# Two PSUM banks of a unit in one VectorE instruction, in a kernel of chunked gated attention and two MLPs

## The chip, the cores and the metric

One core of one Trainium2 chip runs the whole program. The metric is device time in microseconds. Times come from several executions of each kernel; one further execution is profiled.

## The reference

```python
for t in range(S):                       # 768 steps, batch 4, 8 heads, head size 40
    m_new = max(f_gate + m, i_gate)
    f_stab, i_stab = exp(f_gate + m - m_new), exp(i_gate - m_new)
    C = f_stab * C + i_stab * outer(v, k)
    n = f_stab * n + i_stab * k
    denom = max(abs(n . q), 1.0)
    y[t] = sigmoid(o_gate) * (C @ q) / denom
x = y as (3072 tokens, 320)
h = x @ w_in;   x = max(0.01 * h, h) @ w_out        # 320 -> 2048 -> 320
h = x @ w_in2;  out = (h * cos(h)) @ w_out2         # the same sizes
```

All data is float32 in DRAM. The MLP products are made from a rounded high part and a remainder, three matmuls for each product of two.

## The kernel before, in words

The recurrence is cut into **units**: one batch and one chunk of 128 tokens, 24 units in all, each with two sub-chunks of 64. The MLPs go over eight **blocks** of 384 tokens, three units each. The MLPs' hidden layer is 16 tiles wide, and a tile of one block is a **slot** of the program: in it TensorE (PE) makes eight matmuls of 384 columns for the hidden tile (`first_product`, L698) and nine matmuls of 320 columns for the output sums of an earlier tile (`second_product`, L711 to L713). The order of all work is written out by hand. While the first MLP works on block n, the slots also carry the attention work of the three units of block n + 1, at places fixed by the tables `FIRST_SLOTS` and `UNIT_SLOTS` (`SCORES`, `PROBS`, `STATE`, `OUTPUTS`, `READ`, `TURN`, ...). The first three units run before the first slot. In the second MLP no attention work is left.

A unit uses two PSUM banks, one for each half of its heads. After the first three units (which use `s0` and `s1`, then `h0` and `h1`, then `acc0` and `acc1`) these are always `s0` and `s1`. Its path is this:

- PE makes the scores into columns 0 to 255 of both banks (L617).
- VectorE (DVE) multiplies them with the decays `D` (`probs`, L1159; for the first three units `first_probs`, L1168), one instruction for each bank, 128 x 256 each.
- PE makes the unit's own part of the state (`unit_state`, L637). It waits for `P_done` of this unit's probabilities and for `x1_done` of the unit before.
- DVE adds the state up (`state`, L1254 and L1246). GpSimd (POOL) masks it (`own_state`, L1462).
- PE makes the outputs and the sums for the normaliser (`unit_within` L667, `unit_carried` L652).
- DVE makes the normaliser `max(|n.q|, 1)` and its reciprocal (`normaliser`, L1190, L1194, L1197): `max(-x, 1)` and then `max(x, .)`, each in one instruction for each bank, 128 x 4 each, then one reciprocal over all eight heads. `nrm_done` releases POOL, which multiplies the gate with it (`gated`, L1470).
- DVE multiplies outputs and gate (`outputs`, L1227 and L1228 for the last 64 columns, L1231 for all of them, one instruction for each bank, 128 x 160 each). Unit 2 alone has its outputs normalised in PSUM first (`normalised`, L1204).
- PE transposes the result (`unit_transpose`, L674). ACT rounds it (L871) and DVE takes the remainder (`x_lo`, L1264, L1265).

POOL runs in its own written order. For each unit: `gated` of the unit before (L1470), `decay_logs` (L1432), `mask` (L1437), `keys` (L1449), `carried` (L1443), then `own_state` (L1462). So whatever releases L1470 sets the start of the four instructions behind it.

In every slot of the first MLP, DVE also takes the maximum of the leaky ReLU (L1288) and the remainder of the hidden tile (`g_rest`, L1273), which reads two tensors of SBUF. The order on DVE in a slot is: normaliser, probabilities, state, L1288, L1273, outputs, `x_lo`, sigmoid reciprocals (L1150), remainder of a turned block.

During the first block the weights of the first MLP are also loaded and split into high and low parts. ACT rounds (`copy`, L871), DVE or POOL subtracts (DVE L1364; POOL L1526, L1557), and the loads wait for the buffers that these free.

Of the kernel before, what the change touches and what calls it, by code (L numbers as in the profile page):

```python
# [20 lines left out]
F32 = mybir.dt.float32  # L21
F32R = mybir.dt.float32r
ALU = mybir.AluOpType
ACT = mybir.ActivationFunctionType

P = 128
BATCH, HEADS, SEQ, HD = 4, 8, 768, 40
CHUNK = 128
# [4 lines left out]
TILES = BLOCK // P  # L33
DM, FF = HEADS * HD, 2048
# [3 lines left out]
SIDE = HEADS // 2  # L38
PACK, GROUPS = 2, 4
VD = HD + 1  # L40
# [5 lines left out]
BUFS = 3  # L46
# [37 lines left out]
def build(nc, qk, q3, kvo, ig, fg, w1i, w1o, w2i, w2o, out, g_dram, e_dram, x2_dram):  # L84
    ctx = ExitStack()
    with ctx:
        def sb(name, shape, dt=F32):
            return ctx.enter_context(nc.sbuf_tensor(name, shape, dt))

        def bank(name):  # L90
            return ctx.enter_context(nc.psum_tensor(name, [P, 512], F32))

        def sem(name):
            return ctx.enter_context(nc.semaphore(name))
# [18 lines left out]
        D = sb("D", [P, BUFS, SIDE, CHUNK])  # L113
# [34 lines left out]
        m_s = [g_f[0:GH, 0, :], g_f[0:GH, 1, :]]  # L148
        G_s = [t_f[0:GH, 0, :], t_f[0:GH, 1, :]]

        acc = [bank(f"acc{t}") for t in range(TILES)]
        h_bank = [bank("h0"), bank("h1")]
        s_bank = [bank("s0"), bank("s1")]
        x_bank = bank("x")
        ring_bank = h_bank + s_bank

        gates_in = sem("gates_in")
# [423 lines left out]
        def first(b, c):  # L581
            return isinstance(b, int) and b == 0 and c < TILES

        def unit_banks(b, c):
            return (s_bank, h_bank, acc[0:2])[c] if first(b, c) else s_bank

        def scale_bank(c):
            return (h_bank[0], acc[0], x_bank)[c]
# [503 lines left out]
        def _(dve):  # L1092
# [59 lines left out]
            def probs(b, c):  # L1152

                dve.wait_ge(O_done, unit(b, c))
                dve.wait_ge(S_done, unit(b, c) + 1)
                dve.wait_ge(D_done, late(b, c))
                for e in range(2):
                    d = D[:, c % BUFS, 2 * e:2 * e + 2, :]
                    last = tt(d, unit_banks(b, c)[e][:, 0:2 * CHUNK].rearrange("p (h t) -> p h t", h=2), d, ALU.mult)  # L1159
                last.then_inc(P_done, 1)  # L1160

            def first_probs(c):

                dve.wait_ge(S_done, c + 1)
                dve.wait_ge(dx_done, c + 1)
                for e in range(2):
                    d = D[:, c, 2 * e:2 * e + 2, :]
                    last = tt(d, unit_banks(0, c)[e][:, 0:2 * CHUNK].rearrange("p (h t) -> p h t", h=2), d, ALU.mult)  # L1168
                last.then_inc(ph_done, 1)

            def first_keys():

# [4 lines left out]
                   kn_s[:, 0, :, :].rearrange("p (u h) d -> p u h d", u=SUBS), weights.to_broadcast([P, SUBS, SIDE, HD]),  # L1177
                   ALU.mult).then_inc(kw0_done, 1)

            def output_heads(b, c, e):  # L1180
                return unit_banks(b, c)[e][:, OUT:OUT + SIDE * VD].rearrange("p (h d) -> p h d", h=SIDE)

            def normaliser(b, c):

                n, p = unit(b, c), c % 2
                dve.wait_ge(O_done, n + 1)
                sums = [output_heads(b, c, e)[:, :, HD] for e in range(2)]
                parts = [nrm[:, p, SIDE * e:SIDE * (e + 1)] for e in range(2)]
                for o, x in zip(sums, parts):
                    last = ts(x, o, -1.0, 1.0, ALU.mult, ALU.max)  # L1190
                last.then_inc(nrm_step, 1)
                dve.wait_ge(nrm_step, n * 2 + 1)
                for o, x in zip(sums, parts):
                    last = tt(x, o, x, ALU.max)  # L1194
                last.then_inc(nrm_step, 1)
                dve.wait_ge(nrm_step, n * 2 + 2)
                nc.vector.reciprocal(nrm[:, p, :], nrm[:, p, :]).then_inc(nrm_done, 1)  # L1197

            def normalised(b, c):

                dve.wait_ge(nrm_done, unit(b, c) + 1)
                for e in range(2):
                    o, x = output_heads(b, c, e)[:, :, 0:HD], nrm[:, c % 2, SIDE * e:SIDE * (e + 1)]
                    last = tt(o, o, x.unsqueeze(2).to_broadcast([P, SIDE, HD]), ALU.mult)  # L1204
                last.then_inc(normed_done, 1)

            def by_gate(b, c):

# [2 lines left out]
            def outputs(b, c):  # L1211

                p = c % 2
                if by_gate(b, c):
                    dve.wait_ge(gated_done, unit(b, c) + first(b, c))
                else:
                    dve.wait_ge(normed_done, 1)
                    dve.wait_ge(sig_done, 2 * unit(b, c) + 2)
                gate = o_s[:, c % BUFS, :].rearrange("p (h d) -> p h d", h=HEADS)
                if first(b, c):  # L1220
                    if c == 2:
                        dve.wait_ge(T_done, 1)
                else:
                    h, d = divmod(2 * P, HD)
                    n = HD - d
                    o = output_heads(b, c, 1)
                    tt(x1[:, p, DM:DM + n], o[:, h - SIDE, d:HD], gate[:, h, d:HD], ALU.mult)  # L1227
                    tt(x1[:, p, DM + n:DM + REM], o[:, h + 1 - SIDE, 0:HD], gate[:, h + 1, :], ALU.mult)  # L1228
                for e in range(2):
                    heads = slice(SIDE * e, SIDE * (e + 1))  # L1230
                    last = tt(x1[:, p, 0:DM].rearrange("p (h d) -> p h d", h=HEADS)[:, heads, :],  # L1231
                              output_heads(b, c, e)[:, :, 0:HD], gate[:, heads, :], ALU.mult)
                last.then_inc(x1_done, 1)

            def state(b, c):

# [430 lines left out]
```

## Time and profile before

| | us |
|---|---|
| median of 3 runs | 818.16 |
| lowest, highest run | 818.14, 820.23 |
| profiled execution | 818.53 |
| its span, first to last instruction | 816.8 |
| PE busy | 805.9 (99%) |
| DVE busy | 631.1 (77%) |
| ACT busy | 466.6 (57%) |
| POOL busy | 347.2 (43%) |

The granted TensorE clock is 1.00 over the whole span, which is the upper one of its two levels. PE has 6953 matmuls, DVE 1371 instructions. Busy time is a share of the span and says nothing yet of who waits for whom; for that the waits and the timeline are read.

### The profile page before, as it was taken

The page shows a single profiled execution, that of the slowest core. Times are in us where ns is not written, and L with a number is a line of the kernel's source. Part 1 is how long each engine was busy: PE and PEld are TensorE (multiplying, and loading weights), DVE is VectorE, ACT ScalarE, POOL GpSimd, SP SyncE. Part 2 cuts the span into 40 slices and gives each one's busy share as a digit, 9 for nine tenths or more (in the row PEclk, how much of TensorE's full clock was granted, in tenths as well). Part 3 has the DMA queues.
Part 4 walks back from the last instruction along what each step waited for, and adds up shares of the span by engine and source line. Part 5 has one row for each costly group of instructions (what it writes and reads, how often), then busy time and mean ns, then how long its engine had stood idle before and what let it go on. Part 6 is the DMA issues. An engine that isn't in the chain of part 4 may idle for free.

```text
span 816.8 us, 18114 instructions
## 1 busy us (share of the span) xinstructions
PE 805.9 (99%) x6953; PEld 782.8 (96%) x6953; DVE 631.1 (77%) x1371; ACT 466.6 (57%) x1037; POOL 347.2 (43%) x350
## 2 busy tenths in 40 slices
PE   8999999999999999999999999999999999999998
PEld 6888999999999999999999999999999999999998
DVE  8889777776777777777644688888888888888896
ACT  5554433443434334434356777777777777777776
POOL 5877553333343534433126543343434343433332
PEclk9999999999999999999999999999999999999999
DMA  9776243323223333240034401210010202020000
GB/s 288 220 201 195 91 123 105 129 80 129 81 93 131 122 104 128 81 144 31 2 116 127 164 2 49 73 50 25 9 65 1 74 1 73 1 73 1 2 24 25
DMA packets 36952, 70.10 MB, mean 86 GB/s; under 512 B 3524, under 2 KB 24068, under 8 KB 36868
## 3 DMA queue, kind: packets, MB, share of 16 engines
q1 hardware_dynamic: 36820, 68.91, 25.9%
q8 instruction: 55, 0.90, 0.5%
q14 instruction: 29, 0.24, 0.1%
q10 hardware_dynamic: 48, 0.05, 0.0%
HBM read 56.95 MB, written 11.99 MB: 84 GB/s over the span
## 4 chain that ended last, share of the span: by engine, by line
PE 88%; DVE 5%; POOL 2%; ACT 1%; issue 1%; DMA 1%; SPq 0%; DVEq 0%; POOLq 0%; ACTq 0%
PE h L698 32%; PE acc L711 13%; PE acc L713 13%; PE acc L712 12%; PE s L698 10%; PE x L674 2%; PE s L637 2%; PE s L652 2%; DVE r_f L1300 2%; PE s L617 2%; PE s L667 1%; DVE r_f L1298 1%; DMA raw_in<-w1i 1%; DVE g_f L1308 0%; POOL w_in L1526 0%
## 5 line engine op out<-in xcount | busy, mean ns | idle before, releaser
L698 PE MATMUL h<-xT,w_in 128*128 128x384 f32 x1536 | 305.9, 341 | 1.4 <-DVE w_in L1364 0.9
L698 PEld LDWEIGHTS h<-xT,w_in 128*128 128x128 f32 x1536 | 266.3, 188 | 5.5 <-DVE w_in L1364 1.1
L871 ACT ACTIVATE t_f<-h 128x384 f32<-128x384 f32 x192 | 94.1, 490 | 280.7 <-PE h L698 280.6
L711 PE MATMUL acc<-w_out,g_hi 128*128 128x320 f32 x756 | 237.1, 314 | 0.7 <-POOL g_lo L1600 0.3
L713 PE MATMUL acc<-w_out,g_lo 128*128 128x320 f32 x756 | 233.6, 309 | 0.0
L712 PE MATMUL acc<-w_out,g_hi 128*128 128x320 f32 x756 | 232.3, 307 | 0.0
L1600 POOL TENSOR_TENSOR g_lo<-g_f,g_hi 128x384 fp32r<-128x384 f32 x123 | 125.9, 1024 | 204.0 <-ACT g_hi L871 204.0
L1288 DVE TENSOR_TENSOR g_f<-h,t_f 128x384 f32<-128x384 f32 x128 | 71.2, 556 | 107.9 <-ACT t_f L871 107.4
L711 PEld LDWEIGHTS acc<-w_out,g_hi 128*128 128x128 f32 x756 | 142.0, 188 | 2.0 <-issue 1.1
L712 PEld LDWEIGHTS acc<-w_out,g_hi 128*128 128x128 f32 x756 | 142.1, 188 | 0.0
L713 PEld LDWEIGHTS acc<-w_out,g_lo 128*128 128x128 f32 x756 | 141.8, 188 | 0.0
L871 ACT ACTIVATE g_hi<-g_f 128x384 fp32r<-128x384 f32 (+1 forms) x254 | 131.0, 516 | 5.1 <-DVE g_f L1308 4.5
L1300 DVE SCALAR_TENSOR_TENSOR r_f<-t_f,r_f 128x384 f32<-128x384 f32 x127 | 117.7, 927 | 4.4
L698 PE MATMUL s<-xT,w_in 128*128 128x384 f32 x512 | 100.8, 338 | 0.0
L1273 DVE TENSOR_TENSOR g_lo<-g_f,g_hi 128x384 fp32r<-128x384 f32 x128 | 90.9, 710 | 0.0
L698 PEld LDWEIGHTS s<-xT,w_in 128*128 128x128 f32 x512 | 89.7, 188 | 0.0
L1010 ACT ACTIVATE r_f<-r_f,half_pi 128x384 f32<-128x384 f32 x127 | 78.5, 618 | 4.1
L1470 POOL TENSOR_TENSOR kvo_s<-kvo_s,nrm 128x320 f32<-128x320 f32 x23 | 16.6, 723 | 147.9 <-DVE nrm L1197 147.9
L1296 DVE TENSOR_SCALAR t_f<-t_f 128x384 f32<-128x384 f32 x127 | 46.6, 367 | 42.3 <-ACT t_f L871 42.2
L1462 POOL TENSOR_TENSOR Cm<-C,own 80x328 f32<-80x328 f32 x44 | 42.9, 979 | 56.1 <-DVE C L1254 45.2
L1008 ACT ACTIVATE r_f<-r_f 128x384 f32<-128x384 f32 x127 | 65.6, 516 | 0.0
L1150 DVE RECIPROCAL kvo_s<-kvo_s 128x160 f32<-128x160 f32 x48 | 54.9, 1144 | 0.0
(160 smaller groups left out, 834.3 us busy)
## 6 DMA issues: line engine op xcount, KB each, us to landing
qk_s<-qk SPq DMA_DIRECT2D x24, 512.0 KB, 4.7
kvo_s<-kvo SPq DMA_DIRECT2D x24, 484.0 KB, 4.9
x_dram<-stage SPq DMA_DIRECT2D x8, 960.0 KB, 4.2
xT<-x_dram SPq DMA_DIRECT2D x8, 960.0 KB, 4.8
D<-g_dram SPq DMA_DIRECT2D x42, 128.0 KB
qe<-q SPq DMA_DIRECT2D x24, 160.0 KB, 3.2
out<-x SPq DMA_DIRECT2D x24, 160.0 KB, 1.8
eG_b<-e_dram SPq DMA_DIRECT2D x42, 80.0 KB
```

The costliest lines, as they stand in the source:

```text
L698: last = nc.tensor.matmul(bank[:, 0:BLOCK], w(a), x[:, k, :], start=(n == 0), stop=(n == 7))
L711: nc.tensor.matmul(acc[t][:, 0:DM], hi[:, r], w_out[:, 0, j, :], start=(j == 0), stop=False)
L712: nc.tensor.matmul(acc[t][:, 0:DM], hi[:, r], w_out[:, 1, j, :], start=False, stop=False)
L713: nc.tensor.matmul(acc[t][:, 0:DM], lo[:, r], w_out[:, 0, j, :], start=False, stop=(j == FT - 1)).then_inc(out_done, 1)
L871: copy = lambda o, i, **k: nc.scalar.activation(o, i, ACT.Copy, **k)
L1008: nc.scalar.activation(r, r, ACT.Abs).then_inc(fold_done, 1)
L1010: nc.scalar.activation(r, r, ACT.Sin, bias=half_pi[:, 0:1], scale=-1.0).then_inc(sin_done, 1)
L1150: nc.vector.reciprocal(o, o).then_inc(sig_done, 1)
L1273: tt(lo_of(row.tile(i)), g_of(row.tile(i)), hi_of(row.tile(i)).bitcast(F32), ALU.subtract).then_inc(lo_done, 1)
L1288: tt(g_of(row.tile(i)), h_bank[i % 2][:, 0:BLOCK], t_f[:, i % 2, :], ALU.max).then_inc(max_done, 1)
L1300: nc.vector.scalar_tensor_tensor(r, k, -TWO_PI_LO, r, ALU.mult, ALU.add).then_inc(red_done, 1)
L1600: nc.gpsimd.tensor_tensor(lo_of(n), g_of(n), hi_of(n).bitcast(F32), ALU.subtract).then_inc(lo_done, 1)
```

## The change

The PSUM banks of `acc`, `h`, `s` and `x` are declared as tensors of several banks. The old names become views of them, so that PE and ACT address what they addressed before. In `probs`, `first_probs`, `normaliser`, `normalised` and `outputs` the loop over the two banks becomes one instruction whose access pattern has a bank dimension. Waits and increments of semaphores stay the same, and the order of what is left stays the same on every engine.

```diff
-        def bank(name):
-            return ctx.enter_context(nc.psum_tensor(name, [P, 512], F32))
+        def banks(name, n):
+            return ctx.enter_context(nc.psum_tensor(name, [P, n, 512], F32))
...
-        acc = [bank(f"acc{t}") for t in range(TILES)]
-        h_bank = [bank("h0"), bank("h1")]
-        s_bank = [bank("s0"), bank("s1")]
-        x_bank = bank("x")
+        acc_banks, h_banks, s_banks, x_banks = banks("acc", TILES), banks("h", 2), banks("s", 2), banks("x", 1)
+        acc = [acc_banks[:, t, :] for t in range(TILES)]
+        h_bank = [h_banks[:, k, :] for k in range(2)]
+        s_bank = [s_banks[:, k, :] for k in range(2)]
+        x_bank = x_banks[:, 0, :]
...
+        def unit_pair(b, c):
+            return (s_banks, h_banks, acc_banks[:, 0:2, :])[c] if first(b, c) else s_banks
...
-                for e in range(2):
-                    d = D[:, c % BUFS, 2 * e:2 * e + 2, :]
-                    last = tt(d, unit_banks(b, c)[e][:, 0:2 * CHUNK].rearrange("p (h t) -> p h t", h=2), d, ALU.mult)
-                last.then_inc(P_done, 1)
+                d = D[:, c % BUFS, :, :].rearrange("p (e h) t -> p e (h t)", e=2)
+                tt(d, unit_pair(b, c)[:, :, 0:2 * CHUNK], d, ALU.mult).then_inc(P_done, 1)
...
-            def output_heads(b, c, e):
-                return unit_banks(b, c)[e][:, OUT:OUT + SIDE * VD].rearrange("p (h d) -> p h d", h=SIDE)
+            def output_heads(b, c):
+                return unit_pair(b, c)[:, :, OUT:OUT + SIDE * VD].rearrange("p e (h d) -> p e h d", h=SIDE)
...
-                sums = [output_heads(b, c, e)[:, :, HD] for e in range(2)]
-                parts = [nrm[:, p, SIDE * e:SIDE * (e + 1)] for e in range(2)]
-                for o, x in zip(sums, parts):
-                    last = ts(x, o, -1.0, 1.0, ALU.mult, ALU.max)
-                last.then_inc(nrm_step, 1)
+                sums, parts = output_heads(b, c)[:, :, :, HD], nrm[:, p, :].rearrange("p (e h) -> p e h", e=2)
+                ts(parts, sums, -1.0, 1.0, ALU.mult, ALU.max).then_inc(nrm_step, 1)
                 dve.wait_ge(nrm_step, n * 2 + 1)
-                for o, x in zip(sums, parts):
-                    last = tt(x, o, x, ALU.max)
-                last.then_inc(nrm_step, 1)
+                tt(parts, sums, parts, ALU.max).then_inc(nrm_step, 1)
...
-                for e in range(2):
-                    o, x = output_heads(b, c, e)[:, :, 0:HD], nrm[:, c % 2, SIDE * e:SIDE * (e + 1)]
-                    last = tt(o, o, x.unsqueeze(2).to_broadcast([P, SIDE, HD]), ALU.mult)
-                last.then_inc(normed_done, 1)
+                o, x = output_heads(b, c)[:, :, :, 0:HD], nrm[:, c % 2, :].rearrange("p (e h) -> p e h", e=2)
+                tt(o, o, x.unsqueeze(3).to_broadcast([P, 2, SIDE, HD]), ALU.mult).then_inc(normed_done, 1)
...
-                for e in range(2):
-                    heads = slice(SIDE * e, SIDE * (e + 1))
-                    last = tt(x1[:, p, 0:DM].rearrange("p (h d) -> p h d", h=HEADS)[:, heads, :],
-                              output_heads(b, c, e)[:, :, 0:HD], gate[:, heads, :], ALU.mult)
-                last.then_inc(x1_done, 1)
+                tt(x1[:, p, 0:DM].rearrange("p (e h d) -> p e h d", e=2, h=SIDE), output_heads(b, c)[:, :, :, 0:HD],
+                   gate.rearrange("p (e h) d -> p e h d", e=2), ALU.mult).then_inc(x1_done, 1)
```

## Rows read from the trace of the kernel before

**Rows 1.** Waits of PE: waited for, us in total, times, longest us
```profile
PE s L637 <- DVE D L1159: 1.5, 1, 1.5
...
PE h L698 <- DVE w_in L1364: 0.9, 1, 0.9
PE s L637 <- issue: 0.7, 1, 0.7
```

**Rows 2.** Busy time by stretch: length, PE, PEld, DVE, ACT, POOL, PEclk, DMA, GB/s
```profile
100.00:150.00 50.00, 49.98 (x484) 47.97 (x483) 37.16 (x99) 19.88 (x45) 21.92 (x21) 1.00 0.35 118
```

**Rows 3.** DVE's groups by form: out, in, count, busy us, mean ns of one
```profile
L1288 DVE TENSOR_TENSOR g_f<-h,t_f 128x384 f32<-128x384 f32 x128 | 71.2, 556 | 107.9 <-ACT t_f L871 107.4
...
L1159 DVE TENSOR_TENSOR D<-s,D 128x256 f32<-128x256 f32 x42 | 15.7, 415 | 0.2
L1231 DVE TENSOR_TENSOR x<-s,kvo_s 128x160 f32<-128x160 f32 x44 | 11.9, 313 | 0.0
...
L1349 DVE TENSOR_TENSOR g_lo<-g_f,g_hi 128x128 fp32r<-128x128 f32 x3 | 0.9, 289 | 1.0 <-ACT g_hi L871 1.0
```

**Rows 4.** Timeline of two units: start us, us, engine, line, idle before
```profile
118.84 0.55 DVE L1273 TENSOR_TENSOR g_lo<-g_f,g_hi 128x384 fp32r<-128x384 f32 x1
...
118.97 1.57 POOL L1437 TENSOR_TENSOR D<-D,hide 128x512 f32<-128x512 f32 x1
...
207.87 0.23 DVE L1190 TENSOR_SCALAR nrm<-s 128x4 f32<-128x4 f32 x2 [0.49 <-PE s L652]
...
208.69 0.72 POOL L1470 TENSOR_TENSOR kvo_s<-kvo_s,nrm 128x320 f32<-128x320 f32 x1 [8.48 <-DVE nrm L1197]
...
210.48 0.55 DVE L1273 TENSOR_TENSOR g_lo<-g_f,g_hi 128x384 fp32r<-128x384 f32 x1
...
210.57 1.61 POOL L1437 TENSOR_TENSOR D<-D,hide 128x512 f32<-128x512 f32 x1
...
211.15 0.55 DVE L1231 TENSOR_TENSOR x<-s,kvo_s 128x160 f32<-128x160 f32 x2
...
211.84 0.43 PEld L674 LDWEIGHTS x<-ident,x 128*128 128x128 f32 x3
```

**Rows 5.** Timeline of the first block where PE waits for L1159
```profile
26.42 0.56 DVE L1231 TENSOR_TENSOR x<-h,kvo_s 128x160 f32<-128x160 f32 x2
...
27.91 3.58 POOL L1526 TENSOR_TENSOR w_in<-raw_in,w_in 128x768 fp32r<-128x768 f32 x2 [1.52 <-DVE t_f L1128]
...
47.93 0.74 DVE L1159 TENSOR_TENSOR D<-s,D 128x256 f32<-128x256 f32 x2
...
48.73 0.81 PE L637 MATMUL s<-kvo_s,kw 64*80 64x82 f32 x16 [1.47 <-DVE D L1159]
```

**Rows 6.** Timeline of the first block, the two units before PE's wait at 72.9
```profile
58.71 0.20 DVE L1197 RECIPROCAL nrm<-nrm 128x8 f32<-128x8 f32 x1
...
71.29 0.72 POOL L1470 TENSOR_TENSOR kvo_s<-kvo_s,nrm 128x320 f32<-128x320 f32 x1 [1.54 <-DVE nrm L1197]
...
72.26 0.55 DVE L1231 TENSOR_TENSOR x<-s,kvo_s 128x160 f32<-128x160 f32 x2
...
72.91 0.52 PE L637 MATMUL s<-kvo_s,kw 64*80 64x82 f32 x8 [0.66 <-issue]
```

**Rows 7.** L1437 of POOL and L1273 of DVE by source: ns min/median/max
```profile
L1437 POOL TENSOR_TENSOR D<-D,hide x21: 1427/1582/1803, 39.9 to 374.0; 128x512 f32<-128x512 f32 x21
...
L1273 DVE TENSOR_TENSOR g_lo<-g_f,g_hi x128: 543/548/2252, 36.0 to 462.6; 128x384 fp32r<-128x384 f32 x128
```

**Rows 8.** Timeline: POOL begins 0.38 before DVE, and 0.12 before it
```profile
247.25 1.29 POOL L1443 TENSOR_TENSOR qe<-qe,eG_b 80x512 f32<-80x512 f32 x1
...
247.63 1.33 DVE L1273 TENSOR_TENSOR g_lo<-g_f,g_hi 128x384 fp32r<-128x384 f32 x1
...
461.27 1.01 POOL L1545 TENSOR_TENSOR w_in<-raw_in,w_in 128x384 fp32r<-128x384 f32 x1 [0.81 <-ACT w_in L871]
...
461.39 1.31 DVE L1300 SCALAR_TENSOR_TENSOR r_f<-t_f,r_f 128x384 f32<-128x384 f32 x1
```

More of the change, by code:

```diff
@@ L1165, in first_probs @@
                 dve.wait_ge(dx_done, c + 1)
-                for e in range(2):
-                    d = D[:, c, 2 * e:2 * e + 2, :]
-                    last = tt(d, unit_banks(0, c)[e][:, 0:2 * CHUNK].rearrange("p (h t) -> p h t", h=2), d, ALU.mult)
-                last.then_inc(ph_done, 1)
+                d = D[:, c, :, :].rearrange("p (e h) t -> p e (h t)", e=2)
+                tt(d, unit_pair(0, c)[:, :, 0:2 * CHUNK], d, ALU.mult).then_inc(ph_done, 1)
             def first_keys():
@@ L1225, in outputs @@
                     n = HD - d
-                    o = output_heads(b, c, 1)
+                    o = output_heads(b, c)[:, 1]
                     tt(x1[:, p, DM:DM + n], o[:, h - SIDE, d:HD], gate[:, h, d:HD], ALU.mult)
                     tt(x1[:, p, DM + n:DM + REM], o[:, h + 1 - SIDE, 0:HD], gate[:, h + 1, :], ALU.mult)
-                for e in range(2):
-                    heads = slice(SIDE * e, SIDE * (e + 1))
-                    last = tt(x1[:, p, 0:DM].rearrange("p (h d) -> p h d", h=HEADS)[:, heads, :],
-                              output_heads(b, c, e)[:, :, 0:HD], gate[:, heads, :], ALU.mult)
-                last.then_inc(x1_done, 1)
+                tt(x1[:, p, 0:DM].rearrange("p (e h d) -> p e h d", e=2, h=SIDE), output_heads(b, c)[:, :, :, 0:HD],
+                   gate.rearrange("p (e h) d -> p e h d", e=2), ALU.mult).then_inc(x1_done, 1)
             def state(b, c):
```

## The prediction

> **What bounds the kernel now.** I read the waits of PE first, then the busy time by stretch, then the timeline. PE is busy for 99% of the span, and its waits add up to a few microseconds. The larger ones that follow the start-up are three in the first block: 1.5 us for the probabilities of L1159, 0.9 us for a weight split on DVE (L1364), and 0.7 us before L637, which the profile puts down to issue [rows 1]. From 100 us on nothing waits: PE is busy for 49.98 of 50 us while DVE has 37.16 [rows 2], and so it stays to the end of the attention work. The second MLP has none of the changed instructions. So DVE's own time is worth nothing from 100 us on; what counts there is only whether DVE or POOL becomes late enough to stop PE. In the first 100 us, time taken off the chain that ends in one of the three waits is gained one for one, until the wait is used up.
>
> **What the change removes.** For each unit one of two instructions in the probabilities, two of four in the normaliser, one of two in the outputs: 24 x 4 = 96, and one more for unit 2, so 97 of DVE's 1371. PE, ACT, POOL and the transfers issue what they issued. What one merge saves has to be estimated, since no row of before shows an instruction over two banks. DVE's durations give about 1.08 ns for each element: (556 - 313) / 224 between 160 and 384 elements read from PSUM, and (556 - 415) / 128 = 1.10 [rows 3].
> - Outputs: one instruction of 320 elements would take 313 + 160 x 1.08 = 486 ns; the pair takes 0.55 us [rows 4]. Saving 0.06 us.
> - Probabilities: 415 + 256 x 1.10 = 697 ns against 0.74 us for the pair [rows 3, 5]. Saving 0.05 us.
> - Normaliser: the pair of 4 elements takes 0.23 us [rows 4], one of 8 takes hardly more than one of 4. By the pair, the second begins about 0.07 us behind the first. Saving 0.07 us a merge, 0.14 us for the normaliser.
>
> The bounds for one merge: at best nearly half a small pair goes, 0.11 us (0.23 / 2), if each of its instructions costs the same share of it; at worst the two halves no longer overlap, 2 x 415 = 0.83 us against 0.74, which is 0.09 us slower. I take 0.07, since the overlap of the pair is seen in the rows. DVE's busy time should fall by about 24 x (0.05 + 0.14 + 0.06) = 6 us.
>
> The Trainium skill (Perfetto Trace Analysis, section Optimizing Scalar/DVE Operations) gives some 125 ns of overhead to each DVE instruction on PSUM; by that figure the normaliser would save 0.25 us and DVE 12 us.
>
> **What of it lies on a path that sets the end.** Three places.
>
> *The wait at 48.73 (1.47 us).* PE waits for L1159. Followed back, the chain runs over a weight load and POOL's splits to a scan on DVE, which releases POOL's L1526 at 27.91 and stands right behind the outputs of unit 1 [rows 5]. Merges on this chain: the probabilities at 47.93 (0.05), the outputs at 26.42 (0.06), and in front of those about one merge's worth of the earlier probabilities, L1168 (0.05 to 0.07). Sum 0.17 us, all of it out of a wait of 1.47, if the load in the middle takes as long as before.
>
> *The wait at 72.91 (0.66 us).* L637 follows the outputs of the unit before, which end at 72.26 + 0.55 = 72.81 [rows 6]; so the releaser is `x1_done`, not issue. In front of these stands POOL's L1470 at 71.29, released by the normaliser. So this unit's normaliser and outputs count: 0.14 + 0.06 = 0.20. The unit before is on the same path: its normaliser (58.71) starts POOL's chain, which runs without a gap to the split that holds DVE up here; that gives 0.2 again at most, nothing at least. I take 0.35 us of 0.66.
>
> *The wait for L1364 at 82 (0.9 us).* Its chain starts at a hidden tile of PE and holds no merged instruction. Zero; it moves along with PE.
>
> From 100 us on: zero. The cover is DVE's slack of some 13 us in 50 [rows 2] and the fact that after each outputs-and-probabilities pair DVE waits for ACT anyway.
>
> Sum: 0.17 + 0.35 = 0.5 us off the profiled execution's 818.53, so 818.0. That execution lies 0.37 above the median of 818.16, so the forecast against the median is **817.6**. The bounds of the merge, over the same five or so places, give 816.9 to 818.7.
>
> **The rival that makes it slower: the order of POOL and DVE on shared reads flips.** POOL's L1437 takes 1427 ns at least, but 1582 in the median [rows 7], and the long ones end a fixed time after the start of DVE's L1273: 210.57 + 1.61 = 210.48 + 1.70, and 118.97 + 1.57 = 118.84 + 1.70 [rows 4]. In these 14 units, from 101 to 374 us, L1273 begins 0.09 to 0.13 us before L1437, and L1437 stands still until DVE has read. Where POOL is first, DVE stands still: L1273 takes 1.33 us in place of 548 ns and ends 0.42 us after POOL's L1443 [rows 7, 8]. Now L1437 comes 1.88 us behind L1470, which the normaliser releases [rows 4]. With the normaliser 0.14 us shorter, POOL would arrive 0.14 us earlier, that is 0.01 to 0.05 us *before* L1273, whose start hangs on PE and ACT and does not move. If POOL is then served first, L1437 ends at 210.43 + 1.43 = 211.86 and L1273 at 212.28. The outputs ended at 211.15 + 0.55 = 211.70, 0.67 us behind the end of L1273 (211.03); with 0.06 less they would now end at 212.28 + 0.61 = 212.9. The transposes L674, which wait for them, began at 211.84 [rows 4]. PE would stand for 1.08 us in each unit: 14 x 1.08 = +15, so 833. If only the units with the smallest margin flip (about 5), +5.4, so 823.
>
> The Trainium skill (SBUF — State Buffer, section SBUF: two separate sides) says that the pair of ports is held as a lock for a whole instruction and goes to whichever of the two starts first. If the starts are the recorded ones, this rule gives the 833. By the page's 125 ns the lead would even be 0.12 to 0.16 us.
>
> Against it: what counts is the request, not the record's start, and the rows let me work out the difference. DVE reads 384 elements at (548 - 289) / 256 = 1.01 ns, 0.39 us [rows 3, 7], so 0.16 of its 0.55 lies before and behind the read. A delayed L1437 ends 1.15 us after L1273's end; alone it takes 1.43, so 0.28 us is POOL's time before its request plus DVE's time behind the read. The difference, 0.12 us, is by how much POOL's request comes later after its start than DVE's does. So POOL should have to start more than 0.12 us earlier to be first. The one close case agrees: POOL 0.12 us ahead of DVE at 461.3, and DVE is the one delayed, 1.31 us [rows 8]. After the change the lead is 0.05 at most. The turning point is a normaliser that is more than 0.21 us shorter, or 0.105 for each merge, just inside my bound of 0.11. If DVE stays first, L1437's end is pinned to DVE as before, and nothing behind it on POOL moves.
>
> **A second rival: the change does less than it says.** The two-bank instruction takes as long as the pair. Then neither chain moves, and the time is that of before, 818.2; at 0.09 us slower for each it would be 818.7. The rows speak only mildly for it: they have no such access pattern at all.
>
> **A third: more is gained.** When POOL does come out of step in some slots without being in DVE's way, `carried` ends earlier and frees L1273 and then the remainder of the turned unit, for which five transposes of a block wait a little (L674 behind L1265). That is 5 x 0.14 = 0.7 us more, 816.9. It needs L1437 not to be pinned, which the rows contradict.
>
> **Chances.** DVE stays first and the two chains shorten: 0.70, 817.6. The merge gives nothing or a little less than nothing: 0.10, 818.2 to 818.7. More gained: 0.04, 816.9. All 14 units flip: 0.09, 833. Some flip: 0.07, around 823. A measurement of this kernel can tell about 0.3% from no change, 2.5 us here. The first three cases lie within that, 0.84 less a little for what I have overlooked on either side: same 0.82, faster 0.03, slower 0.15. The runs of before themselves reach from 818.14 to 820.23, so the range goes from 816.6 to 820.6; it leaves out the flips.
>
> **What would show it.** In the profile of the changed kernel: DVE with 1274 instructions and about 625 us; L1190's successor 128x8 at about 0.16 us; the outputs at 0.49 and the probabilities at 0.70; POOL's gated product 0.14 us sooner after PE's last L652 matmul. L1273's successor still at 0.55 us and the mask at about 1.7 in those 14 units would show that DVE is first; L1273 at about 1.9 us, and PE waiting at L674 behind the outputs, would show the flip and prove me wrong. The waits at 48.7 and 72.9 should be smaller by 0.2 and 0.35 us; if the first grew, the weight load between has moved.

## The result, and the profile after

The changed kernel takes **828.12 us** in the median of 8 runs (823.67 to 830.52), the kernel before 818.90 beside it (818.08 to 820.83). The ratio is 1.0098, 95% interval 1.0071 to 1.0124: about 1% slower. The forecast was 817.6, range 816.6 to 820.6, so the time lies far above the range. In a later session the same kernel gave 824.32 (822.14 to 828.45), and in a third 824.05 (822.13 to 830.56). Beside each other, its executions spread over 7 us and those of before over 3.

The profiled execution took 828.43 us. The page's header, busy time and granted clock of the kernel after:

```profile
span 826.7 us, 18017 instructions
PE 809.3 (98%) x6953; PEld 785.1 (95%) x6953; DVE 633.1 (77%) x1274; ACT 467.6 (57%) x1037; POOL 345.7 (42%) x350
PEclk9999999999999999999999999999999999999999
```

DVE has 97 instructions fewer and is busy for *longer* than before (631.1). The span has grown by 9.9 us. The lines of the changed instructions, by form (columns: line, engine, operation, names, shapes, count | busy us, mean ns | idle before):

```profile
L1263 DVE TENSOR_TENSOR g_lo<-g_f,g_hi 128x384 fp32r<-128x384 f32 x128 | 97.9, 765 | 0.0
L1162 DVE TENSOR_TENSOR D<-s,D 128x512 f32<-128x512 f32 x21 | 14.3, 681 | 0.2
L1222 DVE TENSOR_TENSOR x<-s,kvo_s 128x320 f32<-128x320 f32 x22 | 10.5, 478 | 0.0
L1190 DVE TENSOR_TENSOR nrm<-s,nrm 128x8 f32<-128x8 f32 x22 | 3.7, 166 | 0.7
L1188 DVE TENSOR_SCALAR nrm<-s 128x8 f32<-128x8 f32 x22 | 3.6, 164 | 9.7 <-PE s L656 9.7
```

The merged instructions are as fast as I estimated or a little faster: 681 ns against 0.74 us for the pair of probabilities, 478 ns against 0.55 for the pair of outputs, and 164 to 166 ns against 0.23 for a pair of the normaliser [rows 4, 5]. All changed instructions together keep DVE busy for 36.2 us, against 42.6 before, which is 0.066 us for each of the 97 merges. So the time was not lost in them. What became longer is an instruction that the change does not touch: `g_rest`, now L1263 and L1273 in the kernel before. Its 128 instances took 90.9 us together there (the page gives 710 ns in the mean) and take 97.9 now. The waits of PE (columns: what waits, for whom, us in total, times, longest) show two places:

```profile
PE s L641 <- DVE D L1162: 4.6, 1, 4.6
PE x L678 <- DVE x L1222: 3.8, 6, 0.6
...
PE s L641 <- issue: 0.3, 1, 0.3
```

The first was 1.5 us, the second is new, the third was 0.7 [rows 1]. To place the difference, I compared when PE starts the scores of each unit (L617 before, L621 after) in the two profiles. After is later than before by 1.32 us at 41 us, by 6.08 at 56 and by 5.69 at 79. From 97 to 387 us it grows in six steps of 0.6 to 0.85 us to 10.0, and then stays. So there are two separate losses: six steps in the attention part, and one piece in the first block.

**The six steps.** This is one of them, from the timeline of after (columns: start, us, engine, line, operation and tiles, count [idle before and releaser]):

```profile
217.62 1.30 POOL L1427 TENSOR_TENSOR D<-D,hide 128x512 f32<-128x512 f32 x1
217.66 1.68 DVE L1263 TENSOR_TENSOR g_lo<-g_f,g_hi 128x384 fp32r<-128x384 f32 x1
...
219.46 0.47 DVE L1222 TENSOR_TENSOR x<-s,kvo_s 128x320 f32<-128x320 f32 x1
...
219.99 0.55 PE L678 MATMUL x<-ident,x 128*128 128x128 f32 x3 [0.63 <-DVE x L1222]
```

And this is the next unit, which has no step:

```profile
235.67 1.70 POOL L1427 TENSOR_TENSOR D<-D,hide 128x512 f32<-128x512 f32 x1
235.68 0.55 DVE L1263 TENSOR_TENSOR g_lo<-g_f,g_hi 128x384 fp32r<-128x384 f32 x1
...
236.34 0.48 DVE L1222 TENSOR_TENSOR x<-s,kvo_s 128x320 f32<-128x320 f32 x1
...
237.22 0.49 PE L678 MATMUL x<-ident,x 128*128 128x128 f32 x3
```

POOL's mask starts 0.04 us before DVE's L1263 in the first case, and 0.01 before it in the second. In the first, POOL runs at its own speed and DVE stands still: 1.68 us in place of 0.55, with an end 0.42 us behind the end of the mask. In the second it is the other way round. I call the first case a flip. It is the rival of the prediction, in 6 of the 14 units. After a flip the outputs are ready late, and PE waits 0.63 us for them.

**The first block.** There the clock fell. Granted clock by microsecond (columns: stretch, its length, busy us of PE, PEld, DVE, ACT and POOL with instructions, granted clock, share of DMA, GB/s):

```profile
37.00:38.00 1.00, 1.00 (x4) 1.00 (x4) 1.00 (x2) 0.65 (x1) 0.92 (x3) 0.50 0.81 211
...
54.00:55.00 1.00, 1.00 (x8) 0.85 (x5) 1.00 (x2) 0.00 (x0) 0.00 (x0) 0.50 0.97 326
```

and PE's timeline there, with the wait that follows:

```profile
34.90 1.57 PE L727 MATMUL x<-ident,stage 32*64 32x16 f32 x48 [0.45 <-ACT stage L918]
36.41 4.61 PE L702 MATMUL h<-xT,w_in 128*128 128x384 f32 x16
...
53.27 1.07 PE L641 MATMUL s<-kvo_s,kw 64*80 64x82 f32 x16 [4.64 <-DVE D L1162]
```

A clock of 0.50 is the lower of the two levels, 1.2 GHz. Two hidden tiles take 4.61 us there, and 3.05 in a later profile of the same kernel (below) with the clock at 1.00. PE loses 1.5 us with it; since it had won 0.2 before, 1.3 are left at 41. Then the wait for unit 3's probabilities has grown by 3.2 us, and behind it the clock is low once more, from 54 to 57 us, for another 1.5 us. The third wait, predicted to shrink by 0.35 us, did: 5.69 in place of 6.08.

### The profile page after: what moved, and what is told of

Read it like the earlier page. It is cut to its first block, busy times and chain, and to the rows that moved or that the text cites. A ratio compares the mean times of both kernels' runs of the same rounds, so it can differ in the third digit from the quotient of the medians.

```text
span 826.7 us, 18017 instructions
## 1 busy us (share of the span) xinstructions
PE 809.3 (98%) x6953; PEld 785.1 (95%) x6953; DVE 633.1 (77%) x1274; ACT 467.6 (57%) x1037; POOL 345.7 (42%) x350
## 4 chain that ended last, share of the span: by engine, by line
PE 86%; DVE 8%; POOL 2%; ACT 2%; issue 2%; DVEq 0%; POOLq 0%; ACTq 0%
PE h L702 31%; PE acc L715 12%; PE acc L717 12%; PE acc L716 12%; PE s L702 10%; PE x L678 2%; PE s L641 2%; PE s L656 2%; DVE r_f L1290 2%; PE s L621 2%; DVE g_lo L1263 1%; PE s L671 1%; DVE r_f L1288 1%; DVE g_f L1278 1%; DVE w_in L1354 1%
## 5 line engine op out<-in xcount | busy, mean ns | idle before, releaser
L1263 DVE TENSOR_TENSOR g_lo<-g_f,g_hi 128x384 fp32r<-128x384 f32 x128 | 97.9, 765 | 0.0
L1452 POOL TENSOR_TENSOR Cm<-C,own 80x328 f32<-80x328 f32 x44 | 41.1, 938 | 63.8 <-DVE C L1244 53.0
```

The costliest lines, as they stand in the source:

```text
L1263: tt(lo_of(row.tile(i)), g_of(row.tile(i)), hi_of(row.tile(i)).bitcast(F32), ALU.subtract).then_inc(lo_done, 1)
```

## The experiments

The kernel before ran beside each group of runs. Its median was 818.35 in the first, 819.81 in the second, 818.32 in the third and 819.91 in the fourth, since nearly all kernels here have two common times some 1.5 to 1.8 us apart; the lowest is always 818.07 to 818.18. So I give lowest times too. `first(b, c)` is true for the first three units. "Pairs" means one instruction for each bank, as before.

**Early or late merges.** Two kernels split the change in time: merged only from unit 3 on, and merged only in the first three units.

```diff
-                ts(parts, sums, -1.0, 1.0, ALU.mult, ALU.max).then_inc(nrm_step, 1)
+                for e in ((0, 1) if first(b, c) else (slice(0, 2),)):
+                    last = ts(parts[:, e], sums[:, e], -1.0, 1.0, ALU.mult, ALU.max)
+                last.then_inc(nrm_step, 1)
```

(and the same in the other merges; in the second kernel the condition is turned round.)

> The first three units keep one instruction for each bank; from unit 3 on everything is in one instruction over both banks. Theory A (the time of the change has two separate sources: about 6 us from the start-up, where the shorter work of the first three units moves the first hidden tile, TensorE's clock falls at 37 us and the wait at 48.7 grows from 1.5 to 4.6 us; and 4.3 us from six units in which GpSimd's mask gets in front of VectorE's remainder): the profile is as before up to 58 us, with granted clock 1.00 at 37 us and a wait near 1.4 us at 48.7; six units still wait at the transposes; 818.2 + 4.3 - 0.4 = about 822. Theory B (one instruction over two banks is bad in itself, wherever it stands): 826 to 828, with no part of it gone. Theory C (everything comes from the first three units): 818.

Measured: 823.11 us (822.15 to 824.41, 6 runs), ratio 1.0052 (1.0037 to 1.0067). Its profile has the six flips, and its clock does not fall in the first block.

```profile
PE x L678 <- DVE x L1233: 3.8, 6, 0.6
...
PE s L641 <- DVE D L1162: 1.4, 1, 1.4
```

> Only the first three units have one instruction over both banks; from unit 3 on there is one for each bank. Theory A: no unit after 100 us waits at the transposes behind the outputs; the clock falls at 37 us in many executions and the wait at 48.7 is 3 to 5 us; 818.2 + 6 = about 824 with a wide scatter. Theory B: about 819. If the clock doesn't fall here, the start-up of the change needs the later merges too, and theory A is wrong in its first half.

Measured: 822.15 us (818.08 to 826.58, 12 runs), ratio 1.0035 (1.0009 to 1.0061). Six executions lie between 818.08 and 819.9, six between 824.4 and 826.58, the latter all with a mean granted clock of 0.995. The profiled one, 826.56, has no flip and this:

```profile
PE s L641 <- DVE D L1163: 4.7, 1, 4.7
```

The two losses are separate: the late merges give the flips in every profile, and the early ones the fallen clock, in some executions.

**The flips taken away by an order.** POOL's mask (from unit 5 on) waits until DVE has finished the instruction in front of L1263. No instruction is left out.

```diff
                 pool.wait_ge(arg_done, late(b, c))
+                if unit(b, c) >= TILES + 2:
+                    n, k = divmod(unit(b, c) - 2 - TILES, TILES)
+                    i = [i for i, s in (UNIT_SLOTS if n else FIRST_SLOTS)[READ].items() if s == k][0]
+                    pool.wait_ge(max_done, n * FT + i + 1 + H_FREE)
                 mask(c)
```

> The change, and one wait more: before each mask GpSimd waits until VectorE has finished the maximum of the hidden tile that stands in front of the remainder, so that the remainder is first again in all units. Theory A: the six waits of TensorE at the transposes are gone (3.8 us of waits in the profile), the mask takes 1.7 us in place of 1.3 in these units, and the time falls by 4.3 us against the change, to about 824; the start-up stays as bad as in the change. Theory B: no difference to the change, 828.

> Both cures together: the first three units with one instruction for each bank, and the wait before the mask. Theory A: both sources are gone and only the small gain at the wait of 72.9 us is left: 817.8, which is the same as before within 0.3%. Theory B: still 824 or more.

Measured: the changed kernel with the order 819.25 us (817.72 to 824.48, 12 runs), ratio 1.0003 (0.9988 to 1.0018); the late merges with the order 819.44 (817.77 to 821.40), ratio 1.0002 (0.9989 to 1.0015). The timeline of the first shows the mask 0.25 us behind DVE:

```profile
211.30 0.55 DVE L1263 TENSOR_TENSOR g_lo<-g_f,g_hi 128x384 fp32r<-128x384 f32 x1
211.55 1.45 POOL L1427 TENSOR_TENSOR D<-D,hide 128x512 f32<-128x512 f32 x1 [0.44 <-DVE g_f L1278]
```

No transposes wait, and the page counts the merges at last without the flips:

```profile
PE 807.2 (99%) x6953; PEld 783.7 (96%) x6953; DVE 623.7 (76%) x1274; ACT 466.6 (57%) x1037; POOL 345.1 (42%) x350
```

DVE: 631.1 - 623.7 = 7.4 us less. Of these, 6.4 lie in the merged instructions. Most of the rest is an instruction that is not changed and stands still less often: `g_rest` takes 90.1 us here and 90.9 before. The flips are the cause of the late loss: the order alone, with every merge kept, removes it. The lowest execution is 0.35 us below that of before, where I had forecast 0.5; the medians can't tell the two kernels apart.

**Which merge flips, and from which lead.** Four kernels: the change once more; only the normaliser merged, everywhere; only the *first step* of the normaliser merged; and, for a larger lead, the change with the normaliser's second step `max(x, .)` left out, so that it makes only `max(-x, 1)`.

```diff
-                ts(parts, sums, -1.0, 1.0, ALU.mult, ALU.max).then_inc(nrm_step, 1)
-                dve.wait_ge(nrm_step, n * 2 + 1)
-                tt(parts, sums, parts, ALU.max).then_inc(nrm_step, 1)
+                ts(parts, sums, -1.0, 1.0, ALU.mult, ALU.max).then_inc(nrm_step, 2)
```

> The change as it is, once more beside the others, since the times scatter by several microseconds and seem to lie on steps. Theory A (two sources: the mask in front of the remainder in six units, and a fall of TensorE's clock at 37 us that draws a long wait and a second fall after it): its times lie on 822.1 (no fall), some 824 (one early fall) and 828 to 830 (the falls at 37 and 54 us), with most of them on the last. If nearly all lie at 822 to 824 here, the start-up part is a matter of chance between executions and not of the change.

> Only the normaliser's two steps are each one instruction over both banks; probabilities and outputs stay one for each bank. The mask then comes 0.14 us earlier, as in the change. Theory A: the same six units wait at the transposes, a little longer each (the outputs are 0.06 us slower), so 822.5 plus what the start-up gives. Theory D (the outputs or probabilities over two banks are what makes TensorE wait): no such wait, 818.

> Only the first of the normaliser's two steps is one instruction over both banks. The mask comes 0.07 us earlier, so it still begins 0.02 to 0.06 us behind the remainder. Theory A: no unit flips, 818.1 at the lowest, and the wait at 72.9 us shrinks by 0.1. If some flip nevertheless, the turning point is not where the recorded starts meet.

> The change, and the second step of the normaliser is left out (the sum's sign is no longer taken off, so the output differs where the sum is positive and above 1); the mask comes another 0.2 us earlier. Theory A: now all 14 units have the mask in front of the remainder; TensorE waits 14 times at the transposes for about 0.5 us and more, and the time rises by about 8 x 0.7 = 5 us over the change, lowest near 827 to 828. If POOL being first is not what costs, the time stays at the change's.

Measured:

| kernel | mask minus L1263 in the 14 units, us | flips | median (lowest) us | ratio |
|---|---|---|---|---|
| before | +0.089 to +0.129 | 0 | | |
| half | +0.023 to +0.060 | 0 | 818.41 (817.99), 12 runs | 0.9994 (0.9984 to 1.0004) |
| change_again | -0.045 to -0.006 | 6 | 824.32 (822.14), 6 runs | 1.0080 (1.0057 to 1.0103) |
| nrm_only | -0.041 to -0.006 | 6 | 824.21 (822.73), 6 runs | 1.0054 (1.0039 to 1.0069) |
| over | -0.130 to -0.174 | 14 | 830.37 (827.90), 4 runs | 1.0146 (1.0118 to 1.0174) |

The starts in this table are those of the traces in nanoseconds, which the timelines round to 0.01 us. Over all profiles the two cases do not overlap: every unit in which POOL is 0.023 us or more ahead is flipped, and none in which it is 0.014 us or less ahead. So POOL is first as soon as its recorded start is some 0.02 us ahead. The flips come with the normaliser's merges alone, and one of its two merges is not enough. With a lead of 0.13 us or more all 14 units flip; one of them, in the timeline of that kernel:

```profile
214.18 1.30 POOL L1425 TENSOR_TENSOR D<-D,hide 128x512 f32<-128x512 f32 x1
214.35 1.55 DVE L1261 TENSOR_TENSOR g_lo<-g_f,g_hi 128x384 fp32r<-128x384 f32 x1
...
216.55 0.55 PE L678 MATMUL x<-ident,x 128*128 128x128 f32 x3 [0.51 <-DVE x L1220]
```

DVE is held up less, since POOL's instruction has run longer when it comes, and the wait is 0.51 in place of 0.63. A flip costs about 0.7 us: the starts of the scores in change_again go from -0.58 us against before at 97 us to +3.77 at 387, 4.35 us for six flips, 0.72 each. In `over` they go from +0.74 to +9.64, 8.9 us for 14 flips, 0.64 each. (Its lowest time of 827.90 is 9.8 above before; its profiled execution, 828.02, was already 1.66 us behind at the scores at 9 us, by the slower third group told of below.)

**The clock in the first block.** The profile of change_again (822.14 us) has no fallen clock. Its rows at the place where it fell in the first profile:

```profile
34.90 1.57 PE L727 MATMUL x<-ident,stage 32*64 32x16 f32 x48 [0.45 <-ACT stage L918]
36.41 3.05 PE L702 MATMUL h<-xT,w_in 128*128 128x384 f32 x16
```

The starts are the same to 0.01 us; the two executions of one program part only within the next instruction. My first theory was that PE's idle time there brings the fall: its wait before L727 is 0.45 us, and 0.18 before. I filled it with products of which nobody uses the result, in the kernel with early merges only and in the ordered one.

```diff
                 if row.starts(0, i) and i == 1:
+                    warm_up(6, acc[2])
                     pe.wait_ge(gate_exp, 4)
```

> Only the first three units have one instruction over both banks, as in the earlier run, and TensorE gets six idle products of 128 columns at the place where it otherwise waits for the gate weights at 34.5 us. Theory A1 (the clock falls at 37 us because the first hidden tile starts 0.5 us earlier and TensorE then waits 0.5 in place of 0.2 us for these weights): the fall is gone in all executions; 818.1 and 819.8 only. Theory A2 (the fall has another cause, such as the order of the start itself): about 4 of 10 executions at 824 and above as before.

> The change with the wait before the mask, and the same six idle products. Theory A1: all executions at 817.7 or, with the slow first matmuls at 7 us, 819.4, none above 820; median about 818, the same as before. Theory A2: one in ten at 824.

Measured: 822.22 us (819.04 to 826.66, 12 runs), ratio 1.0041 (1.0024 to 1.0058), and 821.79 (820.14 to 826.68, 11 runs), ratio 1.0025 (1.0014 to 1.0035). Both profiled executions were late ones (826.55 and 826.60). Their clock does not fall at 37 us, but the wait for the probabilities is long again, and it is during this wait, at 51.8 and 52.5 us, that the clock falls, for 10 us. From the profile of first_warm:

```profile
39.06 3.04 PE L702 MATMUL h<-xT,w_in 128*128 128x384 f32 x16
```

```profile
50.00:58.00 8.00, 5.23 (x44) 4.65 (x46) 7.96 (x16) 1.46 (x3) 5.49 (x6) 0.61 0.73 207
```

```profile
PE s L641 <- DVE D L1164: 3.1, 1, 3.1
```

The filling moved the loss and did not remove it. It also made the hidden tiles 0.65 us later than in first_only (39.06 against 38.41), which is a loss of its own. The idle time before L727 is not the whole cause. And since the clock stood at 1.00 when this wait began, the long wait does not need a fallen clock ahead of it; what it does need is read below, with the rows of the first block.

The change without the normaliser's merges, and the kernel before once more beside them:

> Everything over both banks but the normaliser, which keeps one instruction for each bank. Theory A: the mask comes as in the kernel before and no unit flips; the probabilities and outputs are 0.06 us shorter each, which moves the waits in the first block by about 0.2 us; the first hidden tile starts somewhat earlier; 817.9 at the lowest, without waits at the transposes. If units flip here, the outputs or the probabilities move the mask after all.

> The kernel before, unchanged, under another name and profiled once more: whether its second step of time (819.8 to 820.3) shows in the profile. Expected: the first matmuls at 7 us take 2.0 us in place of 1.1 and everything behind them is 1.5 to 1.8 us later, or not, with nothing else different.

Measured: 819.14 us (818.00 to 820.28, 12 runs), ratio 1.0003 (0.9993 to 1.0012), no flip and no late execution; and 819.94 (818.25 to 821.57, 10 runs) for before. Despite its label, the latter is the kernel before without an edit, and tells nothing of the filling. Its profile shows where the two common times come from, at the third group of matmuls of the program:

```profile
6.89 2.05 PE L803 MATMUL acc<-t_f,x 128*128 128x128 f32 x8 [1.13 <-DVE t_f L1128]
8.87 1.81 PE L812 MATMUL acc<-x,stage 128*64 128x256 f32 x8
```

In the profile of before that the prediction used, the same two groups take less:

```profile
6.89 1.13 PE L803 MATMUL acc<-t_f,x 128*128 128x128 f32 x8 [1.12 <-DVE t_f L1128]
7.95 1.08 PE L812 MATMUL acc<-x,stage 128*64 128x256 f32 x8
```

The granted clock is printed as 1.00 here in both, but that is no reading: the trace's first clock record, which is of the upper level, begins at 6.07 us in the one with 1.13 and at 10.39 in the one with 2.05. The 1.00 given for the whole span of before holds from 6.07 us on. In all 18 profiles the two go together: eight take 1.13 us and their record begins at 4.8 to 6.3 us, ten take 2.04 or 2.05 and it begins at 10.0 to 11.5. Single matmuls of 128x128 at 2 us, before any record, take 421 ns in both profiles; at 7 us they take 275 ns in the one and still 421 in the other. So the two common times differ by when the upper level is granted. Why it comes later in some executions stays open.

**Which early merge brings the late executions.** A last group, all on one chip: the change a third time, the normaliser merged in the first three units only, probabilities and outputs merged in the first three units only, and the ordered kernel with the first three normalisers in pairs.

```diff
-                for e in ((slice(0, 2),) if first(b, c) else (0, 1)):
+                for e in (0, 1):
```

> The changed kernel once more, beside three others on the same chip, since its share of executions with a fallen clock was 7 of 8 in one session and 2 of 6 in another. Every theory has its lowest executions at about 822.1 (six flipped units). Chip theory (how often the clock falls hangs on the chip, not on the edit): whatever share it shows, the other three kernels show nearly the same. Edit theory: a third or more of its 12 executions at +4 to +6 (clock 0.997 or lower).

> Only the normaliser of the first three units over two banks (6 merges), all else as before. Normaliser theory (the fall of the clock near 37 us is brought by the shorter normaliser of these three units): a third or more of the executions at about 824 to 827 with clock 0.997 or lower, the rest at 818.1 to 820; median 819 to 824. Other-merge theory (it is brought by probabilities and outputs): all executions at 818 to 820.5. Chip theory: the same share as the changed kernel beside it.

> Only the probabilities and outputs of the first three units over two banks, the normaliser in pairs, all else as before. Normaliser theory: no execution with a fallen clock, 818 to 820.5. Other-merge theory: a third or more at 824 to 827. Chip theory: the same share as the changed kernel beside it. Both merges needed together: none in this kernel nor in the one with the normaliser alone.

> The changed kernel with the ordering wait before the mask and with the normaliser of the first three units in pairs. Normaliser theory: no flip and no fallen clock, so lowest 817.7 and median 817.7 to 819.4, against 818.1 and 818.3 to 819.8 of before, that is 0.4 us faster at best. Other-merge theory: as above with some executions at 824. Chip theory: the same share of fallen clocks as the changed kernel beside it.

Measured: change_third 824.05 us (822.13 to 830.56, 6 runs), ratio 1.0082 (1.0051 to 1.0114); first_nrm 818.35 (818.12 to 823.10, 12 runs), 1.0005 (0.9991 to 1.0019); first_rest 819.75 (from 818.13; 12 runs, of which two took 2336 and 2488 us and count in neither the ratio nor the table below), 1.0004 (0.9994 to 1.0014); ordered_split 818.51 (817.67 to 823.50, 12 runs), 0.9999 (0.9981 to 1.0016). None of the theories on record for these four holds alone. I count an execution as late when it is 4 us or more above the lowest of its kernel, over all sessions:

| first three units | kernels | PE's wait before L727 (L723), us | late executions |
|---|---|---|---|
| everything merged | change (9 of 20), over (2 of 4), first_only (6 of 12), ordered (1 of 12), first_warm (4 of 12), ordered_warm (2 of 11) | 0.45 to 0.63, none where filled | 24 of 71 |
| the normaliser alone, or all but the normaliser | ordered_split (2 of 12), first_nrm (2 of 12), first_rest (0 of 10), nrm_split (0 of 12), nrm_only (0 of 6) | 0.31 to 0.32 | 4 of 52 |
| pairs, or one step of the normaliser | late_only (0 of 6), late_ordered (0 of 12), half (0 of 12), before (1 of 124) | 0.17 to 0.24 | 1 of 154 |

What follows: the early merges together make late executions more common than pairs do. In the group with first_only and ordered, all on one chip, 7 of 24 were late with them, 0 of 18 with early pairs and late merges, and 1 of 29 of the kernel before. That a part of the merges makes fewer late executions than all of them is only suggested: beside each other on one chip it was 4 of 34 against 2 of 6. Whether a given execution is late is not set by the program, as the two profiles of the change show. Why the clock falls in one and not in the other stays open, and the table mixes chips, so its shares are rough (the ordered kernel, which is the same program as the change up to 60 us, had 1 of 12 where the change had 5 of 8 in its first session).

## Why the prediction was wrong, point by point

**The step that failed: the 0.12 us between start and request.** The leads that I forecast, POOL "0.01 to 0.05 us before L1273", were measured at 0.005 to 0.045. I then argued from fixed pieces before and behind the read that POOL must start more than 0.12 us earlier to be first, with "the one close case" at 461.3 us as support [rows 8]. The measured turning point lies between 0.014 and 0.023 us. The 0.12 came from a sum of small remainders of durations, and the term that spoiled it is "alone it takes 1.43". That was the shortest L1437 in the kernel before, but it wasn't alone: it, too, stood behind L1273 and ended 1.16 us after it. In all 44 flips of these runs the mask, now really first, takes 1.28 to 1.31 us, and one row of before had hinted at it: L1443 at 247.25, also of 512 elements and first, takes 1.29 [rows 8]. With 1.30 in place of 1.43 the same sum gives 1.30 - 1.15 - 0.16 = -0.01 us, so that POOL would be first as soon as the starts meet. This is worked out afterwards, but the measured point is close to it. The supporting case was another pair of instructions, and it supported nothing: a POOL that starts 0.12 us ahead is first with a turning point of 0.12 and with one of 0.02. The rule of the Trainium skill (SBUF — State Buffer, section SBUF: two separate sides), that the ports go to whichever of the two starts first, I had set aside for this working; the runs agree with it to 0.02 us in the recorded starts.

**The rival's size.** "If only the units with the smallest margin flip (about 5), +5.4, so 823": 6 flipped, and the executions without a fallen clock begin at 822.13. The price of a flip was 1.08 us in the prediction and is 0.7. A part of the difference is one misread row: 211.84 is the weight load of the transposes [rows 4], and their matmuls begin 0.18 us behind it:

```profile
212.02 0.49 PE L674 MATMUL x<-ident,x 128*128 128x128 f32 x3
```

A second part is again the mask, 1.43 us in the sum and 1.30 in a flip. Without these two, 1.08 becomes 0.77; measured in change_again were steps of 0.84 or 0.85 in three of the six units and of 0.62 in the others; I have not traced this difference. For all 14 units I said 833; the kernel in which all flip has its lowest execution at 827.90.

**The first block, not foreseen.** I counted the early merges as 0.17 us gained before 48.73. In change_again PE's work at 41 us is 0.24 earlier than before, and 0.28 at 56: somewhat more than forecast, and mostly won earlier than at the wait I named, which went from 1.47 to 1.4. But some executions come out late. The profiled one was 6.1 us behind at 56 us, the larger part of the 9.9. How the long wait comes about can be followed in the rows. In change_again, where it is short, the pair of POOL's `carried` (L1433) and DVE's `g_rest` has DVE first:

```profile
42.34 0.61 DVE L1263 TENSOR_TENSOR g_lo<-g_f,g_hi 128x384 fp32r<-128x384 f32 x1
42.49 1.61 POOL L1433 TENSOR_TENSOR qe<-qe,eG_b 80x512 f32<-80x512 f32 x1
```

In after POOL is 0.5 us earlier and DVE 0.9 later:

```profile
41.97 2.00 POOL L1433 TENSOR_TENSOR qe<-qe,eG_b 80x512 f32<-80x512 f32 x1
43.21 3.72 DVE L1263 TENSOR_TENSOR g_lo<-g_f,g_hi 128x384 fp32r<-128x384 f32 x1
43.93 1.57 POOL L1547 TENSOR_TENSOR w_out<-raw_out,w_out 128x640 fp32r<-128x640 f32 x1
45.46 1.06 POOL L1422 TENSOR_TENSOR D<-D,colb 128x512 f32<-128x512 f32 x1
...
48.72 1.59 POOL L1433 TENSOR_TENSOR qe<-qe,eG_b 80x512 f32<-80x512 f32 x1
49.11 3.50 DVE L1354 TENSOR_TENSOR w_in<-raw_in,w_in 128x768 fp32r<-128x768 f32 x1
50.27 1.52 POOL L1547 TENSOR_TENSOR w_out<-raw_out,w_out 128x640 fp32r<-128x640 f32 x1
...
52.53 0.68 DVE L1162 TENSOR_TENSOR D<-s,D 128x512 f32<-128x512 f32 x1
```

DVE's `g_rest` comes behind POOL's start, is held up by three of POOL's instructions one after the other, and takes 3.72 us in place of 0.61. This is the larger part of the delay. Then DVE's remainder of the weights is held up by two more and takes 3.5 us (1.81 in change_again), and the probabilities stand behind it. It is again an order of DVE and POOL that has turned, and it goes with the long wait in every profile. In 14 of the 18, DVE is 0.15 us ahead at this pair, its instruction takes 0.60 or 0.61 us, and the wait is 1.39 to 1.47. In the other four (after, first_only, first_warm, ordered_warm) POOL is 1.24 us ahead, DVE's instruction takes 2.70 to 3.72 us, and the wait is 3.04 to 4.70.

What makes DVE late for this pair differs. In after and first_only the hidden tiles had run at the low clock. In first_warm and ordered_warm they had run at the upper one, and were late because the filling stood in front of them. So the fallen clock is one way into this loss, and no necessary one. That the lateness of the tiles is what turns the pair is my reading of these rows. No run held the order at this place, so it isn't shown that holding it would take the loss back.

**What was right.** The merge: forecast 0.05 to 0.07 us each and 6 us in all, measured 0.066 and 6.4 in the changed instructions. The Trainium skill (Perfetto Trace Analysis, section Optimizing Scalar/DVE Operations), by whose figure DVE would save 12 us, is farther off. The wait at 72.91: forecast -0.35, measured -0.39 (from -0.28 at 67 us to -0.67 at 79 in change_again). From 100 us on, zero without the flips: the ordered kernel is 1.20 us later than before at 67 us (it has the slower third group), 0.81 at 79 and 0.86 at 97. The sum of 0.5: change_again is 0.58 ahead at 97 us, before its first flip. And DVE's 625 us became 623.7 once the flips were gone. The lowest times of the two ordered kernels, 817.67 and 817.72, are near the forecast of 817.6, though their medians, 818.51 and 819.25, can't be told from before.

**The chances.** The forecast had 0.15 for slower and 0.16 for the two flip cases. With leads of 0.01 to 0.05 us on one side and a turning point worked out to a tenth of a microsecond on the other, the two cases should have had equal weight.

## What to carry to other kernels

Where two engines hold each other up, as DVE and POOL do here, and one starts a tenth of a microsecond behind the other in every iteration, a shorter instruction in front of the later one can turn the order round and cost far more than it saves; list such pairs with their leads before you shorten anything. If the order matters, write it down as a wait: it cost nothing here that the runs can tell, and it took away 4 us. A merge over two PSUM banks saved 0.05 to 0.07 us on DVE here, which is worth having only on a path that PE waits for.

## What the runs showed of the hardware that I had not expected

- A lead of POOL of 0.014 us or less in the recorded starts leaves DVE at 0.55 us, and one of 0.023 to 0.045 puts it at 1.68 us, for the same instruction. The loser waits for the whole instruction of the other: DVE's end is 0.42 us behind POOL's when POOL is first.
- One instruction over two banks takes 681 ns for 512 elements and 478 for 320, where my estimates from single-bank rows were 697 and 486, and 164 for 8. There is no extra cost at the bank's edge that these rows show.
- Two executions of one program agreed in their starts to 0.01 us at 36.4 us, and then two hidden tiles took 3.05 us in the one and 4.61 in the other, with granted clocks of 1.00 and mostly 0.50.
- The upper level of TensorE's clock is on record from 4.8 to 6.3 us in eight profiles and only from 10.0 to 11.5 us in the other ten, and eight small matmuls at 6.9 us take 1.13 and 2.05 us with it. This gives nearly every kernel here two common times, some 1.5 to 1.8 us apart.
- DVE's `g_rest` can be held up by a row of POOL's instructions, and not by one alone: 3.72 us in place of 0.61 behind three of them.
